# Three block programs of TensorE in another order, an early count and one wait less in a fused attention and mixture-of-experts kernel

## The chip, the cores and the metric

The kernel runs on one core of a Trainium2 chip. Its time is the time of one execution on the device in microseconds (us); where several runs are given, it is their median.

## What is computed

A chain of three parts on 3072 tokens (4 sequences of 768) with 512 features:

```python
# 1. decayed linear attention, 8 heads of 64, per sequence
state = gamma * state + outer(k[t], v[t]);  y[t] = scale * q[t] @ state
# 2. top-1 mixture of 8 experts, 512 -> 1024 -> 512
e_idx = argmax(x @ w_gate + modality_bias[modality_id])
out[mask] = gate_w[mask, None] * (relu(x[mask] @ w1[e]) @ w2[e])
# 3. bilinear part
h = (x @ w1) * (x @ w2) @ w3
result = h @ w_out
```

## The kernel before, in words

The program of each engine is written out by hand, and the engines meet through counting semaphores. Large products are made from a high and a low half of each operand: every product is three matmuls (helper on L400: high x high, high x low, low x high). ScalarE writes the high half, VectorE subtracts it from the source to get the low half.

There are three stages. The attention stage runs over 24 units (6 chunks of 128 rows in 4 sequences). Beside its end and behind it, w3 and w_out are multiplied into one matrix `wc` (eight products of 24 matmuls, `w3_product`), while VectorE sorts the tokens by expert into tiles of 128 places and writes small tables.

The expert stage works on blocks of one, three or four tiles of one expert. Each engine runs a loop of 13 passes (`each_window`): it loads the number of blocks from `num_tab` once, and in each pass compares it with the pass number; in a pass without a block it does nothing more. TensorE then loads the block's size from `win_tab` and runs one of three programs: `wide(4)` and `wide(3)` (8 hidden products of 12 matmuls, 4 outward products of 24, and two groups of 8 transposes of the next block's rows, with 512 or 384 columns) or `one_tile` (24 + 8 + 24 + 16 + 4 matmuls and transposes). Each program is in the code once. With this input there are eight blocks, of 4, 3, 3, 3, 4, 4, 4 and 1 tiles. POOL gathers the rows, SyncE loads the next expert's weights as soon as the present ones have been split.

`s_hlo` counts the low halves of the hidden layer that VectorE has written. A hidden product f of block w waits until it has reached 8w + f + 1, because its bank is free then. So that the first two products of block 0 may start, VectorE gives two counts by `dve.sem_inc(s_hlo, 2)` on L1383, behind the last piece of `wc` (`wc_lo(7)`) and just ahead of its own block loop. `s_wclo` counts the pieces of `wc` that are lowered; the banks of the outward products hold such pieces earlier.

The last stage, behind the loop, is six groups of 288 matmuls: two products with w1 and w2, and one with `wc`.

Of the kernel before, what the change touches and what calls it, by code (L numbers as in the profile page):

```python
# [32 lines left out]
def build(nc, q_t, k_t, k, v, mod_id, w_gate, mod_bias, we1, we2, wa, wb, w3_t, w_out, out):  # L33
# [9 lines left out]
    KF = FF // P  # L43
# [56 lines left out]
    with ctx:  # L100
# [127 lines left out]
        def sem(name):  # L228
            return ctx.enter_context(nc.semaphore(name))
# [48 lines left out]
        s_wclo = sem("s_wclo")  # L278
# [17 lines left out]
        s_hlo = sem("s_hlo")  # L296
# [48 lines left out]
        def each_window(eng, body):  # L345

            total = eng.value_load(num_tab[0:1, 1:2], min_val=MINW, max_val=NW)
            with eng.Fori(0, NW) as w:
                with eng.If(total > w):
                    body(w, total)  # L350

        def table(eng, w, col, lo, hi):

            at = win_tab[0:1, w:w + 1, col:col + 1] if isinstance(w, int) else win_tab[0:1, bass.ds(w, 1), col:col + 1]
            return eng.value_load(at.rearrange("p a b -> p (a b)"), min_val=lo, max_val=hi)  # L355
# [21 lines left out]
        def early_chunks(f):  # L377

            return (f - 3,) if 3 <= f < 3 + KD else ()
# [415 lines left out]
        def _(pe):  # L795
# [134 lines left out]
            def x_rows(w, chunks):  # L930
                pe.wait_ge(s_xin, w * (16 * GT) + 16 * GT)
                for k in chunks:
                    if not (isinstance(w, int) and w == 0):
                        pe.wait_ge(s_ixlo, w * KD + (k - 1))
                    for t in range(GT):
                        i = pe.transpose(bank[x_bank(w, k)][:, t * P:(t + 1) * P], xin[:, t, k * P:(k + 1) * P], ident)  # L936
                    i.then_inc(s_ixp, 1)

            def hidden(w, run, n, f):
                pe.wait_ge(s_hlo, w * KF + (f + 1))  # L940
                for k in range(KD):
                    if f == 0:
                        pe.wait_ge(s_ixlo, w * KD + (k + 1))
                        pe.wait_ge(s_w1lo, run * KD + (k + 1))
                    i = product(pe, bank[f % 2][:, 0:n], lambda a: we1_p[:, a, k, f * P:(f + 1) * P], lambda a: xT[:, a, k, 0:n],
                                k == 0, k == KD - 1)
                i.then_inc(s_hp, 1)

            def outward(w, run, n, d):
                pe.wait_ge(s_y, w * KD + (d + 1))  # L950
                for f in range(KF):
                    if d == 0:
                        pe.wait_ge(s_hlo, w * KF + (f + 3))
                        if f % 2 == 0:
                            pe.wait_ge(s_w2lo, run * (KF // 2) + (f // 2 + 1))
                    i = product(pe, bank[4 + d % 2][:, 0:n], lambda a: we2_p[:, a, f, d * P:(d + 1) * P], lambda a: hT[:, a, f, 0:n],
                                f == 0, f == KF - 1)
                i.then_inc(s_yp, 1)

            def window(w, total):  # L960
                def wide(tiles):
                    run = table(pe, w, RUN_OF, 0, E - 1)
                    n = tiles * P
                    for f in range(KF):
                        hidden(w, run, n, f)
                    for d in range(KD):
                        outward(w, run, n, d)
                        if d < KD // 2:
                            with pe.If(total > w + 1):
                                x_rows(w + 1, range(2 * d, 2 * d + 2))  # L970
# [29 lines left out]
                    i.then_inc(s_yp, KD - 1)  # L1000

                size = table(pe, w, SIZE, 1, GT)
                with pe.If(size > 3):
                    wide(4)
                with pe.If(size < 4):
                    with pe.If(size > 1):
                        wide(3)
                    with pe.If(size < 2):
                        one_tile()

            def first_x():
                x_rows(0, range(KD))
# [12 lines left out]
                if f == 3:  # L1025
                    token_of_place()
            pe.wait_ge(s_tab, 1)
            pe.wait_ge(s_wclo, KF - 2)
            each_window(pe, window)
            pe.wait_ge(s_wclo, KF)  # L1030

# [32 lines left out]
        def _(dve):  # L1064
# [23 lines left out]
            def lower(pair, raw, sm_):  # L1088
                tt(pair(LO), raw, pair(HI).bitcast(F32), ALU.subtract).then_inc(sm_, 1)  # L1089

            def w1_lo(run, chunks=range(KD)):
                for c in chunks:
                    dve.wait_ge(s_w1hi, run * KD + (c + 1))
                    lower(lambda a: we1_p[:, a, c, :], we1_raw[:, c, :], s_w1lo)
# [67 lines left out]
            def wc_lo(f):  # L1162
                dve.wait_ge(s_wchi, f + 1)
                tt(wc[:, LO, f, :], bank[wc_bank(f)][:, :], wc[:, HI, f, :].bitcast(F32), ALU.subtract).then_inc(s_wclo, 1)  # L1164
# [90 lines left out]
            wide = [1, E, E]  # L1255
# [7 lines left out]
            wide = [1, n_tab, E]  # L1263
# [42 lines left out]
            wide = [1, NG, n_tab]  # L1306
# [12 lines left out]
            w1_lo(0, early_chunks(4))  # L1319
            wc_lo(5)  # L1320
            w1_lo(0, early_chunks(5))
            wc_lo(6)
            w1_lo(0, early_chunks(6))
            x_lo(0, range(KD))
# [55 lines left out]
                with dve.If(total > w + 1):  # L1380
                    x_lo(w + 1, range(KD))

            dve.sem_inc(s_hlo, 2)  # L1383
            each_window(dve, window)


# [63 lines left out]
```

## Time and profile before

| | |
|---|---|
| median of three runs | 878.25 us |
| lowest, highest | 874.43, 881.44 us |
| profiled execution, its own time | 881.25 us |
| its span, first to last instruction | 879.5 us |
| mean granted clock of TensorE | 0.987 |
| TensorE busy in the span | 855.1 us |

The profiled execution's own time is 1.75 us longer than its span. Busy times of the other engines are far smaller (VectorE 283.7, ScalarE 236.2, POOL 89.5 us) and mostly lie beside TensorE's.

### The profile page before, as it was taken

The page shows a single profiled execution, that of the slowest core. Times are in us where ns is not written, and L with a number is a line of the kernel's source. Part 1 is how long each engine was busy: PE and PEld are TensorE (multiplying, and loading weights), DVE is VectorE, ACT ScalarE, POOL GpSimd, SP SyncE. Part 2 cuts the span into 40 slices and gives each one's busy share as a digit, 9 for nine tenths or more (in the row PEclk, how much of TensorE's full clock was granted, in tenths as well). Part 3 has the DMA queues.
Part 4 walks back from the last instruction along what each step waited for, and adds up shares of the span by engine and source line. Part 5 has one row for each costly group of instructions (what it writes and reads, how often), then busy time and mean ns, then how long its engine had stood idle before and what let it go on. Part 6 is the DMA issues. An engine that isn't in the chain of part 4 may idle for free.

```text
span 879.5 us, 14619 instructions
## 1 busy us (share of the span) xinstructions
PE 855.1 (97%) x5722; PEld 733.0 (83%) x5723; DVE 283.7 (32%) x493; ACT 236.2 (27%) x382; POOL 89.5 (10%) x111
## 2 busy tenths in 40 slices
PE   9999999998999999999987999999999999999995
PEld 8899888787999988888876888888888888888884
DVE  3577698521221432111414430230230220220210
ACT  1334433321222432121334331231221221221210
POOL 2222002210102020202000001001001001001001
PEclk9999999999999999999997999999999999999998
DMA  9999881432022042303045002002002001001000
GB/s 332 330 327 306 295 314 48 147 108 83 26 71 96 9 182 95 96 0 96 31 160 156 1 2 95 1 6 90 0 14 81 0 28 68 0 8 41 1 12 37
DMA packets 43093, 83.36 MB, mean 95 GB/s; under 512 B 7345, under 2 KB 7985, under 8 KB 43057
## 3 DMA queue, kind: packets, MB, share of 16 engines
q1 hardware_dynamic: 33376, 60.08, 20.0%
q0 software_dynamic: 4736, 14.72, 5.2%
q10 hardware_dynamic: 4946, 8.08, 2.5%
q8 instruction: 24, 0.39, 0.2%
q14 instruction: 11, 0.09, 0.0%
HBM read 62.64 MB, written 20.22 MB: 94 GB/s over the span
## 4 chain that ended last, share of the span: by engine, by line
PE 93%; DVE 3%; issue 2%; ACT 1%; ACTq 1%; POOL 0%; DVEq 0%
PE bank L400 46%; PE attn L400 33%; PE bank L831 3%; PE attn L858 3%; PE pair L843 3%; PE pair L936 1%; PE bank L870 1%; PE attn L849 1%; PE bank L808 1%; PE bank L1019 1%; DVE w3T L1089 0%; PE pair L815 0%; ACTq L355 0%; DVE wc L1164 0%; DVE we_p L1089 0%
## 5 line engine op out<-in xcount | busy, mean ns | idle before, releaser
L400 PE MATMUL bank<-yT,wab 128*128 128x512 f32 x1152 | 265.1, 392 | 3.4 <-issue 3.4
L400 PEld LDWEIGHTS bank<-yT,wab 128*128 128x128 f32 x1152 | 218.2, 190 | 49.2 <-issue 3.6
L400 PE MATMUL bank<-xT,we_p 128*128 128x512 f32 (+1 forms) x672 | 140.6, 370 | 4.9 <-issue 3.8
L400 PE MATMUL attn<-hT,we_p 128*128 128x512 f32 (+1 forms) x672 | 141.8, 368 | 0.0
L400 PEld LDWEIGHTS bank<-xT,we_p 128*128 128x128 f32 x672 | 123.3, 190 | 21.7 <-issue 6.2
L400 PEld LDWEIGHTS attn<-hT,we_p 128*128 128x128 f32 x672 | 121.3, 188 | 14.4
L400 PE MATMUL attn<-wc,gT 128*128 128x512 f32 x576 | 131.5, 389 | 0.0
L400 PEld LDWEIGHTS attn<-wc,gT 128*128 128x128 f32 x576 | 108.1, 188 | 22.5
L1390 DVE TENSOR_TENSOR g<-bank,acopy 128x512 f32<-128x512 f32 x48 | 33.2, 691 | 255.0 <-PE bank L400 255.0
L1335 DVE SCALAR_TENSOR_TENSOR hT<-bank,hT 128x512 fp32r<-128x512 f32 x56 | 38.7, 690 | 151.5 <-ACT hT L661 151.5
L587 ACT ACTIVATE gT<-g 128x512 fp32r<-128x512 f32 x48 | 30.3, 632 | 137.6 <-DVE g L1390 137.6
L661 ACT ACTIVATE hT<-bank 128x512 fp32r<-128x512 f32 x56 | 33.5, 599 | 103.0 <-PE bank L400 103.0
L574 POOL DMA_INDIRECT out_dram<-otile,row_id x24 | 23.2, 968 | 372.0 <-ACT otile L587 372.0
L587 ACT ACTIVATE acopy<-bank 128x512 f32<-128x512 f32 x48 | 28.7, 598 | 68.1 <-PE bank L400 68.1
L587 ACT ACTIVATE yout<-attn 128x512 f32<-128x512 f32 x29 | 17.3, 597 | 110.0 <-PE attn L400 109.2
L1089 DVE TENSOR_TENSOR gT<-g,gT 128x512 fp32r<-128x512 f32 x48 | 33.2, 692 | 34.4 <-ACT gT L587 34.4
L587 ACT ACTIVATE otile<-attn,meta_in 128x512 f32<-128x512 f32 x24 | 16.5, 689 | 100.0 <-PE attn L400 100.0
L1108 DVE TENSOR_TENSOR prob<-bank,maskt 128x512 f32<-128x512 f32 x48 | 30.9, 685 | 24.2 <-PE bank L831 24.1
L1089 DVE TENSOR_TENSOR xT<-pair,xT 128x512 fp32r<-128x512 f32 x30 | 19.3, 685 | 52.4 <-ACT xT L587 52.4
L1089 DVE TENSOR_TENSOR we_p<-we_raw,we_p 128x1024 fp32r<-128x1024 f32 x24 | 28.3, 1221 | 21.1 <-ACT we_p L587 20.9
L549 POOL DMA_INDIRECT xin<-x_rows,x_id x32 | 31.5, 984 | 11.1 <-issue 7.3
L587 ACT ACTIVATE xTu<-attn 128x512 f32<-128x512 f32 x24 | 14.4, 598 | 59.4 <-PE attn L858 59.4
(168 smaller groups left out, 609.2 us busy)
## 6 DMA issues: line engine op xcount, KB each, us to landing
we_raw<-in_moe_w_dram SPq DMA_DIRECT2D x6, 2048.0 KB, 8.9
yT_sorted<-yout ACTq DMA_DIRECT2D x7, 1024.0 KB, 4.4
qkv<-in_q_t_dram SPq DMA_DIRECT2D x24, 256.0 KB, 3.6
qkv<-in_v_dram SPq DMA_DIRECT2D x24, 256.0 KB, 5.0
x_rows<-x_keep SPq DMA_DIRECT2D x24, 256.0 KB, 3.6
ytile<-yT_sorted SPq DMA_DIRECT2D x6, 1024.0 KB, 5.3
qkv<-in_k_t_dram SPq DMA_DIRECT2D x23, 256.0 KB, 4.7
qkv<-in_k_dram SPq DMA_DIRECT2D x20, 256.0 KB, 5.2
```

Of the source, the lines that this page charges most:

```text
L400: i = pe.matmul(out_, left(a), right(b), start=(first and n == 0), stop=(last and n == 2), **kw)
L549: pool.indirect_dma_start(xin[:, t, :], None, x_rows[:, :], bass.IndirectOffsetOnAxis(ap=x_id[:, t:t + 1], axis=0)).then_inc(s_xin, 16)
L574: pool.indirect_dma_start(out[:, :], bass.IndirectOffsetOnAxis(ap=row_id[:, n:n + 1], axis=0), otile[:, n % 2, :], None).then_inc(s_out[n ...
L587: copy = lambda o, i, **kw: act.activation(o, i, ACT.Copy, **kw)
L661: act.activation(hT[:, HI, f, :], bank[f % 2][:, :], ACT.Relu).then_inc(s_hhi, 1)
L831: i = pe.matmul(bank[2 + r][halves(a), j * P:(j + 1) * P], qkv[head_rows(r), b, KT, keys], qkv[head_rows(r), b, QT, j * P:(j + 1) * P], st ...
L843: i = pe.matmul(pair[halves(a), j, 0:XW], xTu[:, b % 2, j, halves(a)], iw[:, j, :], start=True, stop=True, skip_group_check=True)
L858: i = pe.matmul(attn[out_rows(j, r), r, j // 2 * P:(j // 2 + 1) * P], qkv[:, b, V, h * D:(h + 1) * D], prob[:, b % 2, r, j, :], start=(fir ...
L1089: tt(pair(LO), raw, pair(HI).bitcast(F32), ALU.subtract).then_inc(sm_, 1)
L1108: i = tt(prob[:, u % 2, r, :, :], bank[2 + r][:, :].rearrange("p (j t) -> p j t", j=HP), maskt[:, r, :, :], ALU.mult)
L1335: dve.scalar_tensor_tensor(hT[:, LO, f, :], bank[f % 2][:, :], 0.0, hT[:, HI, f, :].bitcast(F32), ALU.max, ALU.subtract).then_inc(s_hlo, 1)
L1390: tt(g32[:, f % 2, :], bank[2 + f % 2][:, :], acopy[:, f % 2, :], ALU.mult).then_inc(s_g, 1)
```

## The change

Three edits. TensorE's three block programs stand in the code as one tile, three tiles, four tiles, where they stood as four, three, one. VectorE gives the two first counts of `s_hlo` behind the third early chunk of w1, ahead of `wc_lo(6)`. TensorE doesn't wait for six lowered pieces of `wc` ahead of its block loop. The instructions in each program are the same.

```diff
                 size = table(pe, w, SIZE, 1, GT)
+                with pe.If(size < 4):
+                    with pe.If(size < 2):
+                        one_tile()
+                    with pe.If(size > 1):
+                        wide(3)
                 with pe.If(size > 3):
                     wide(4)
-                with pe.If(size < 4):
-                    with pe.If(size > 1):
-                        wide(3)
-                    with pe.If(size < 2):
-                        one_tile()
...
             pe.wait_ge(s_tab, 1)
-            pe.wait_ge(s_wclo, KF - 2)
             each_window(pe, window)
...
             wc_lo(5)
             w1_lo(0, early_chunks(5))
+            dve.sem_inc(s_hlo, 2)
             wc_lo(6)
...
-            dve.sem_inc(s_hlo, 2)
             each_window(dve, window)
```

On TensorE, the entry of the block loop. Before, in program order; `num_tab` holds the number of blocks, `win_tab` the sizes, and the first COMPARE_AND_BRANCH of L1003 asks whether the size is above 3:

```order
L347 TENSOR_LOAD num_tab [waits s_wclo,s_tab]
L347 ISA x2
L348 UNCONDITIONAL_BRANCH
L349 COMPARE_AND_BRANCH
L355 ISA
L355 TENSOR_LOAD win_tab
L355 ISA x2
L1003 COMPARE_AND_BRANCH
...
L943 ISA [waits s_hlo]
L944 ISA [waits s_ixlo]
L400 MATMUL bank<-xT,we_p 128x512 [waits s_w1lo]
```

The same place in the changed kernel, where L1003 asks whether the size is below 4 and L1004 whether it is below 2:

```order
L347 TENSOR_LOAD num_tab [waits s_tab]
...
L355 TENSOR_LOAD win_tab
L355 ISA x2
L1003 COMPARE_AND_BRANCH
L1004 COMPARE_AND_BRANCH
...
L977 ISA [waits s_hlo]
L978 ISA [waits s_ixlo]
L400 MATMUL bank<-we_p,xT 128x512 [waits s_w1lo]
```

Straight behind the compares stood the four-tile program; now the one-tile program stands there, and a block of four tiles branches at L1003 over it and over the three-tile program.

On TensorE, the end of the four-tile program. Before, with the start of the three-tile program behind it:

```order
L400 MATMUL attn<-hT,we_p 128x512 [waits s_y]
L400 MATMUL attn<-hT,we_p 128x512 x23
L1003 UNCONDITIONAL_BRANCH
L1005 COMPARE_AND_BRANCH
L1006 COMPARE_AND_BRANCH
```

In the changed kernel, with the back edge of the loop and the first matmul of the last stage behind it:

```order
L400 MATMUL attn<-hT,we_p 128x512 [waits s_y]
L400 MATMUL attn<-hT,we_p 128x512 x23
L348 REGISTER_ALU
L348 COMPARE_AND_BRANCH
L400 MATMUL bank<-yT,wab 128x512 [waits s_yTlo,s_walo,s_wclo]
```

The four-tile program was followed by the other two; now it is the last one, and the loop's end stands right behind it. The programs of 208 + 76 matmuls between them are passed at another place.

## Rows read from the trace of the kernel before

**Rows 1.** The page: span, and TensorE's busy time and share.
```profile
span 879.5 us, 14619 instructions
...
PE 855.1 (97%) x5722; PEld 733.0 (83%) x5723; DVE 283.7 (32%) x493; ACT 236.2 (27%) x382; POOL 89.5 (10%) x111
```

**Rows 2.** Waits of PE: who waited for whom, us in total, times, longest.
```profile
PE bank L400 <- issue: 7.2, 3, 3.5
...
PE bank L400 <- DVEq L1383: 0.9, 1, 0.9
```

**Rows 3.** The chain in 148 to 165: start us, us, what.
```profile
158.56 0.04 DVE wc L1164
...
158.83 6.18 PE bank L400 x26
```

**Rows 4.** Timeline, 139 to 186, VectorE and SyncE: start, us, engine, operation.
```profile
151.95 0.68 DVE L1164 TENSOR_TENSOR wc<-attn,wc 128x512 fp32r<-128x512 f32 x1
...
152.55 1.21 DVE L1089 TENSOR_TENSOR we_p<-we_raw,we_p 128x1024 fp32r<-128x1024 f32 x1
...
155.67 0.39 SPq L469 DMA_DIRECT2D we_raw<-in_moe_w_dram  x1
...
156.61 1.28 DVE L1089 TENSOR_TENSOR xT<-pair,xT 128x512 fp32r<-128x512 f32 x2
```

**Rows 5.** Timeline of PE where blocks 1, 2, 4 and the last stage begin.
```profile
207.95 8.25 PE L400 MATMUL bank<-xT,we_p 128*128 128x384 f32 x37 [3.53 <-issue]
...
245.12 1.14 PE L400 MATMUL bank<-xT,we_p 128*128 128x384 f32 x5 [0.28 <-issue]
...
316.25 1.09 PE L400 MATMUL bank<-xT,we_p 128*128 128x512 f32 x4
...
475.20 6.99 PE L400 MATMUL bank<-yT,wab 128*128 128x512 f32 x17 [3.35 <-issue]
```

**Rows 6.** The page's DMA queues: packets, MB, share of 16 engines.
```profile
q8 instruction: 24, 0.39, 0.2%
```

**Rows 7.** Queues in stretches from 163.2, 201.3, 204.8, 242.8, 525.6, 553.8, 0.2 us each.
```profile
q8 instruction: 1, 0.02, 30.0%
...
q8 instruction: 1, 0.02, 39.3%
...
q8 instruction: 1, 0.02, 31.6%
...
q8 instruction: 1, 0.02, 41.3%
...
q8 instruction: 1, 0.02, 44.2%
...
q8 instruction: 1, 0.02, 39.0%
```

**Rows 8.** Queues in 243 to 480: the only one of kind instruction.
```profile
q14 instruction: 1, 0.01, 0.0%
```

**Rows 9.** The chain in 200 to 209.
```profile
199.89 4.53 PE attn L400 x20
```

**Rows 10.** Windows: stretch, length, busy us of each engine, PEclk, DMA share, GB/s.
```profile
0.00:50.00 50.00, 47.89 (x924) 44.01 (x927) 24.45 (x55) 11.66 (x20) 13.03 (x21) 1.00 0.94 330
...
155.00:158.00 3.00, 2.90 (x13) 2.06 (x11) 2.89 (x5) 0.07 (x1) 2.39 (x3) 1.00 0.42 63
158.00:165.00 7.00, 6.17 (x27) 5.14 (x28) 1.38 (x2) 1.53 (x3) 2.82 (x4) 1.00 1.01 409
...
207.95:211.60 3.65, 3.65 (x12) 3.65 (x13) 0.00 (x0) 0.00 (x0) 0.00 (x0) 0.54 0.25 95
...
475.20:481.20 6.00, 6.00 (x14) 4.74 (x15) 1.46 (x2) 0.46 (x2) 1.15 (x1) 0.50 0.59 160
```

**Rows 11.** Timeline of PE in the attention stage, at two breaks.
```profile
35.76 0.55 PE L831 MATMUL bank<-qkv 64*64 64x128 f32 x10 [0.20 <-issue]
...
41.07 1.09 PE L858 MATMUL attn<-prob,qkv 128*64 128x128 f32 x16 [0.33 <-issue]
```

## The prediction

> **What bounds the kernel now.** The page comes first: TensorE (PE) is busy 855.1 of 879.5 us [rows 1]. So only PE's idle time, and time at a low clock, can change the end. The table of waits says where PE is idle: 7.2 us in three pieces put down to "issue" (nothing that the profile shows), and 0.9 us put down to VectorE's semaphore instruction on L1383 [rows 2]. The reader should see that the change touches exactly these: L1383 is the early count that is moved, and two of the three issue pieces stand at the block programs whose order is changed.
>
> The place of the 0.9 us: the last w3 product ends at 157.9, ScalarE copies its bank, VectorE starts the subtraction at 158.56, and only then issues the count; PE starts block 0 at 158.83 [rows 3], 0.9 us after its last matmul. The wait that is removed (six wc pieces lowered) was long met: the sixth subtraction of wc began at 151.95 and took 0.68 us [rows 4].
>
> The issue pieces: reading PE's rows at the borders of the eight blocks, block 1 (three tiles) starts at 207.95 after 3.53 us of issue, block 2 (three tiles) after 0.28 us, and block 4 (four tiles) with none; blocks 3, 5, 6 and 7 are like block 4 [rows 5]. 475.20 is the start of the last stage, 3.35 us after the loop. So a three-tile program costs 3.53 us the first time and next to nothing the second. What differs is that its code was new to PE. The transfers of kind "instruction" say the same: the queue q8 moved 24 packets of 0.39 MB in all, 16 KB each [rows 6]. One lies at 201.3 to 201.5 and one at 204.8 to 205.0, around the 3.53 us; from 243 to 480, through five blocks and the exit, q8 moves nothing at all, and the one row of that kind is q14's [rows 7, 8]. I read this as: code comes in pieces of 16 KB, the next piece is fetched ahead while PE goes straight on, a jump to a piece that isn't there waits for its transfer, and pieces once fetched stay for this loop.
>
> How much is a piece? In the last stage, straight-line code, packets start at 525.6 and 553.8 [rows 7]. With 4.53 us for 20 matmuls [rows 9], 0.227 us each, 28.2 us is 124 matmuls with their weight loads. By the code, the four-tile and the three-tile program have 208 matmuls each (96 + 96 and 16 transposes) (1.7 pieces), the one-tile program 76 (0.6). In the kernel before, PE runs the four-tile program straight through, then skips the three-tile and the one-tile programs, 2.3 pieces, to the loop's end: the first such jump lands beyond the piece fetched ahead. That is the stall at 204.42.
>
> **The change, part by part.** All sums are against the profiled execution, 881.25 us for a span of 879.5; the median of the three runs is 878.25, and I carry the difference over to it.
>
> Removed at the first border: with the order one tile, three tiles, four tiles, the end of the four-tile program is followed by the loop's end, and the piece after it is fetched ahead. Block 1 then jumps back to the head and skips only the one-tile program, 0.6 of a piece, which was fetched ahead when PE came to the head. The stall of 3.53 us goes. With it goes a slow stretch: the granted clock is 0.54 over the 3.65 us behind the idle time, nearly all of it at 1.2 GHz [rows 10]; 0.46 x 3.65 is 1.7 us. Together 5.2 us. What is late next there: the path from one block to the next, which the borders after it show as 0.28 us or hidden.
>
> Added at the entry: block 0 has four tiles. PE's sequencer now passes the head, finds size above 3 and jumps over the one-tile and three-tile programs, 2.3 pieces, to code that nobody has fetched. The same kind of stall as at 204.42 is due here, with the same sort of matmul (512 columns) running ahead of it. Its price has four parts. The row of it, 3.53 us. The entry also loads the number of blocks, ahead of the jump: a border without a fetch takes at least from 242.8, where the sequencer is at the loop's end, to the start at 245.12, 2.3 us, for two table loads and the branches; less one empty pass (3.35 us for five at the exit, 0.67; the loop has 13 passes for 8 blocks) leaves 0.8 per load; some of it stands against the back edge that the entry doesn't have, so I take 0.4, between 0 and 0.8. Third, the DMA engines: at 201 they were nearly free, and the two packets there stand 3.5 us apart; in the attention stage, with the engines busy 94% [rows 10], PE came to a fresh piece at 35.76 and again at 41.07, each time after a short issue gap in the middle of its straight-line work [rows 11], so a fetch took up to 5.3 us there, 1.8 more. At the entry the DMA share is 0.42 in 155 to 158 and 1.01 after 158, when the weights of the second expert run stream in; I take 0.7, between 0 and 1.8. The stall is 4.6 us (3.5 to 6.1), and block 0 starts near 162.5. Fourth, the clock: 1.7 us again by the nearest row; the exit's stall was followed by 6.0 us at 0.50, worth 3.0 [rows 10], which is the upper bound.
>
> The early count: VectorE gives it behind the third chunk of w1, which starts at 152.55 and takes 1.21 [rows 4], so from 153.8 on. VectorE spends nothing on it, and nothing queues behind it. The 0.93 us disappear as a wait on VectorE, but the gain is real only to the extent that the new stall does not cover it; I count the stall from 157.90, so 0.93 is taken off whole. Other counts that PE needs (w1 chunks, x pieces) are in by 157.9, the end of the last two x pieces [rows 4]. The removed wait: nothing, as shown; under a fetch of code it could only matter if PE's sequencer had come before 152.6. The PE path at the exit: block 7 has one tile, and its program now stands first, so two more compares are passed before the loop's end; five empty passes of at least three such instructions cost 0.67 each, so two compares are at most 0.4 and I take 0.2. They are not hidden, since PE is idle there. The four-tile blocks pass one branch less, within the lead.
>
> Sum: 4.6 + 1.7 + 0.2 - 0.93 - 3.53 - 1.7 = +0.3 us. The stall changes its place and hardly its size. Bounds: +0.3 - 1.1 - 0.2 = -1.0 and +0.3 + 1.5 + 1.3 + 0.2 = +3.3. That gives 881.6 for an execution like the profiled one and **878.6** against the median.
>
> **Rivals.**
> Hidden fetch: the four-tile program is there when PE jumps, or comes while the w3 products still run. For it: PE's sequencer is some microseconds ahead of its array (the packet at 201.3 begins 3 us before the last matmul of block 0 ends). Against it: the same lead stood before the stall of 3.53 us and did not hide it. It gives -0.93 - 3.53 - 1.7 + 0.2 = -6.0, so 872.3. Chance 10%.
>
> Late fetch, the slower side: the new fetch queues behind the 2 MB of expert weights that are issued at 155.67 [rows 4]. For it: the code packet of block 0 in the kernel before starts only at 163.2 [rows 7], in the middle of that load. If the demanded piece starts there too: at the border PE resumed 6.5 us after the packet's start (201.4 to 207.95), of which the head's branches and the size load, some 2 us by the prices above, lie ahead of the jump here. So PE resumes near 163.3 + 4.5 = 167.8, a stall of 9.9 instead of 4.6: +5.3, so 883.9. It decides against the kernel once the packet starts later than about 157.7, where the stall is 4.3 us. Against it: PE should be at the jump near 156, and the engines are half free until 158. Chance 12%.
>
> Both stalls: the piece with the head or the three-tile program is lost, and the border at block 1 stalls as before. That adds 5.2 to the sum, so 883.8. Against it: the head's piece survived the fetches up to 242.8 in the kernel before [rows 7], since block 2 came back to it for 0.28 us. The Trainium skill has a rule that leads here (Runtime: NRT & Kernel Launch, Instruction fetch mechanics): a taken branch whose target isn't in the current two pages of 16 KB forces a fetch. By that rule every border, in both kernels, would stall; the trace does not agree, with 0.28 us at 245.12, nothing at 316.25, and no code packet in 237 us [rows 5, 8]. Chance 5%.
>
> Not code at all: the 3.53 us belong to something that the order of the programs doesn't touch. Then only the early count acts, at most -0.9, so 877.4. The two packets beside the stall speak against it. Chance 5%.
>
> **How the numbers follow.** The forecast has 68%; its own range, with the bounds above and the spread of a median (the three runs lie 7 us apart), is 875 to 882.5. The range for 8 in 10 reaches half into the cases on each side: 873.5 to 883.5. A measurement of this kernel tells about 1%, 8.8 us, from no change. No single case moves that far: late fetch and both stalls together would. So faster 0.02, within 1% 0.94, slower 0.04.
>
> **What would show it.** In the changed profile: PE idle of 3.5 to 6 us put down to issue ahead of the first matmul of block 0, near 162; a code packet near 157 to 158.5; a clock near one half behind it; no idle of 3.5 us ahead of block 1; the wait on VectorE's count gone from the table; the idle time of the exit at 3.4 to 3.7 us. Block 0 starting by 158 proves the hidden fetch; a start past 165 proves the late one.

## The result, and the profile after

| | before | changed |
|---|---|---|
| median, 20 runs of each | 878.49 us | 882.96 us |
| lowest, highest | 874.34, 881.44 us | 880.32, 887.05 us |
| profiled execution, its own time | 881.25 us | 882.88 us |
| its span | 879.5 us | 881.2 us |

The ratio is 1.0055 with a 95% interval of 1.0042 to 1.0069. The changed kernel is 4.5 us slower, between 3.7 and 6.1. The time lies in the range given for 8 in 10 (873.5 to 883.5) and within 1% of before, but above 882.5, where the forecast case itself ended. The likeliest time was 878.6, and the missing 4.4 us are no chance: the interval leaves the ratio 1 out.

The page of the changed kernel, to be read against [rows 1, 6]: span, busy times and the queue of kind instruction.

```profile
span 881.2 us, 14618 instructions
...
PE 853.3 (97%) x5722; PEld 732.3 (83%) x5723; DVE 283.9 (32%) x493; ACT 236.1 (27%) x382; POOL 88.5 (10%) x111
...
q8 instruction: 26, 0.43, 0.2%
```

There are 26 code packets, two more than before. The waits of PE, against [rows 2]:

```profile
PE bank L400 <- issue: 7.2, 2, 4.4
...
PE bank L400 <- DVE wab L1088: 3.9, 1, 3.9
```

The count's wait on VectorE is gone. The sum put down to issue is 7.2 us again, which looks like no change, but it is now two pieces and the exit's idle time stands in the other row: before, 7.2 was 3.53 + 0.28 + 3.35. The exit's row names VectorE's piece of `wab`, but PE doesn't wait for it: that piece ends 3.67 us behind the last block's end in both traces, and before PE had started at 3.35. Where the pieces stand, on the timeline of PE (against [rows 5]):

```profile
160.34 23.68 PE L400 MATMUL bank<-xT,we_p 128*128 128x512 f32 x96 [2.86 <-issue]
...
207.41 4.35 PE L400 MATMUL bank<-xT,we_p 128*128 128x384 f32 x24
212.24 12.78 PE L400 MATMUL bank<-xT,we_p 128*128 128x384 f32 x72 [0.48 <-DVE hT L1335]
...
247.83 19.23 PE L400 MATMUL bank<-xT,we_p 128*128 128x384 f32 x96 [4.38 <-issue]
```

The same matmuls of blocks 0, 1 and 2 before:

```profile
158.83 22.05 PE L400 MATMUL bank<-xT,we_p 128*128 128x512 f32 x96 [0.93 <-DVEq L1383]
...
207.95 18.47 PE L400 MATMUL bank<-xT,we_p 128*128 128x384 f32 x96 [3.53 <-issue]
...
245.12 17.09 PE L400 MATMUL bank<-xT,we_p 128*128 128x384 f32 x96 [0.28 <-issue]
```

Block 0 starts after 2.86 us, block 1 with none (before: 3.53), and block 2 after 4.38 us (before: 0.28). The 0.48 us inside block 1 are new too: ScalarE comes from a four-tile block, its copy `hT` lies at 210.86, and VectorE and PE follow it.

That these are waits for code can be read from the records of PE's sequencer (the part of the engine that reads the code and hands the matmuls on). The compare-and-branch instructions of the block programs, first before (L1005), then in the changed kernel (L1003 at the entry, L1008 ahead of block 2), with shortest, median and longest time in ns:

```profile
L1005 PEldq COMPARE_BRANCH  x2: 73/2030/3988, 200.2 to 206.1; - x2
```
```profile
L1003 PEldq COMPARE_BRANCH  x1: 3800/3800/3800, 155.2 to 155.2; - x1
...
L1008 PEldq COMPARE_BRANCH  x1: 3896/3896/3896, 240.2 to 240.2; - x1
```

One branch takes 4.0 us before, and two take 3.8 and 3.9 us in the changed kernel; no other branch of PE takes over 0.35 us in either. Each of the three is a jump over programs that aren't run, and each stands ahead of one of the three stalls (3.53, 2.86 and 4.38 us).

Windows behind the two stalls, with the columns of [rows 10]:

```profile
160.34:164.50 4.16, 4.16 (x11) 3.33 (x12) 0.00 (x0) 0.00 (x0) 0.80 (x1) 0.59 1.02 407
...
243.44:247.83 4.39, 0.01 (x2) 0.01 (x1) 0.00 (x0) 0.60 (x1) 0.00 (x0) 0.80 0.63 173
247.83:251.50 3.67, 3.67 (x11) 3.67 (x12) 0.00 (x0) 0.00 (x0) 0.00 (x0) 0.50 0.23 86
251.50:254.00 2.50, 2.50 (x12) 2.50 (x12) 0.69 (x1) 0.60 (x1) 0.00 (x0) 0.73 0.00 0
```

The number behind the five busy times of a row is the granted clock. Behind the entry it is 0.59 over 4.16 us, by the clock alone 0.41 x 4.16 = 1.7 us; behind block 2's stall it is 0.50 and then 0.73, 1.8 + 0.7 = 2.5 us. The matmuls themselves lost a little less: the first 96 of block 0 took 23.68 us against 22.05 (1.6), those of block 2 took 19.23 against 17.09 (2.1), and those of block 1 before took 1.4 more than those of block 2. The stalls of code stand beside packets. Queues in stretches from 155.9 (0.3 us long), 241.7 (0.2) and 246.8 (0.3), against [rows 7]; a packet is counted in the stretch in which it starts, and its share gives how long it took, 0.306 x 16 x 0.3 = 1.47 us for the first:

```profile
q8 instruction: 1, 0.02, 30.6%
...
q8 instruction: 1, 0.02, 30.2%
...
q8 instruction: 1, 0.02, 24.0%
```

They start at 156.17, 241.74 and 246.93 and take 1.47, 0.96 and 1.15 us. The first two lie inside the two long branches (155.22 to 159.02 and 240.18 to 244.07). The third isn't over when PE's matmuls go on at 247.83, so block 2 didn't wait for it. Before, the two last packets of the block loop started at 231.9 and 242.9, and no stall of over 0.3 us stood beside them.

The sum of the two profiled spans, +1.7 us, goes so: attention and w3 stages -0.4; entry +1.9 idle and +1.6 clock; border of block 1 -3.53, -1.4 clock and +0.48; border of block 2 +4.1 idle (4.38 - 0.28) and +2.1 clock; exit +0.57; the one-tile block -2.6 and the last stage -1.3; the rest +0.2. The one-tile block's term is put down to this pair of executions and not to the change: the clock fell there in this one of the kernel before, and didn't in this one of the changed kernel. The same holds for the last stage, where the granted clock over the first 6 us was 0.50 before [rows 10] and 0.72 after. The stretches from the last block's start to its end, before and then after:

```profile
452.21:471.85 19.64, 15.80 (x61) 11.91 (x59) 10.69 (x12) 11.27 (x16) 0.00 (x0) 0.83 0.40 145
```
```profile
457.23:474.26 17.03, 13.15 (x61) 10.00 (x59) 9.80 (x12) 11.19 (x16) 0.00 (x0) 1.00 0.31 109
```

Without those two the spans differ by +5.6 us, against +4.5 between the medians.

### The profile page after: what moved, and what is told of

Its sections match the earlier page's. It is cut to its first block, busy times and chain, and to the rows that moved or that the text cites. A ratio compares the mean times of both kernels' runs of the same rounds, so it can differ in the third digit from the quotient of the medians.

```text
span 881.2 us, 14618 instructions
## 1 busy us (share of the span) xinstructions
PE 853.3 (97%) x5722; PEld 732.3 (83%) x5723; DVE 283.9 (32%) x493; ACT 236.1 (27%) x382; POOL 88.5 (10%) x111
## 4 chain that ended last, share of the span: by engine, by line
PE 92%; DVE 3%; issue 2%; ACT 1%; ACTq 1%; POOL 0%; DVEq 0%
PE bank L400 46%; PE attn L400 32%; PE bank L831 3%; PE attn L858 3%; PE pair L843 3%; PE pair L936 1%; PE bank L870 1%; PE attn L849 1%; PE bank L808 1%; ACTq L355 1%; PE bank L1019 1%; DVE w3T L1088 0%; PE pair L815 0%; ACT wab L587 0%; ACT yout L587 0%
## 5 line engine op out<-in xcount | busy, mean ns | idle before, releaser
L400 PE MATMUL bank<-xT,we_p 128*128 128x512 f32 (+1 forms) x672 | 143.1, 374 | 7.9 <-issue 7.2
L400 PEld LDWEIGHTS bank<-xT,we_p 128*128 128x128 f32 x672 | 125.3, 193 | 25.2 <-issue 8.6
```

Of the source, the lines that this page charges most:

```text
L400: i = pe.matmul(out_, left(a), right(b), start=(first and n == 0), stop=(last and n == 2), **kw)
```

## The experiments

Two theories stood against each other. **The hole** (mine, formed from the result) supposes this: PE's code comes in pieces of 16 KB, some 256 instructions, and the next piece is fetched ahead when PE enters a new one. A jump to a piece that wasn't asked for stalls and leaves the pieces between unfetched. When PE later runs through them, they are fetched, and those behind them once more; if PE then jumps again before a piece is back, it stalls a second time. **The rival**: the second stall belongs to something else in the changed kernel (the early count, the missing wait, the data path from a four-tile to a three-tile block), or to where the programs stand in sequence, whatever the pieces.

Counted in the built programs, in pieces of 256 instructions, the positions are these:

```
                 loop's head   programs in order                   loop's end
before           9.95          four -11.72, three -13.50, one      14.20
changed          9.95          one -10.65, three -12.42, four      14.19
```

At the entry the changed kernel jumps from 9.95 to 12.42. By the theory piece 11 has not been fetched, nor asked for. Block 1 then runs through 10 and 11 and jumps from 12.42 to the end in 14: that is the border of the 4.38 us.

The stages of each profiled execution in us, as far as they matter here ("entry" is the idle time ahead of block 0, "exit" that ahead of the last stage, "q8" the number of code packets, "border" the largest idle time of PE put down to issue ahead of block 1 or 2). The ratio is to the kernel before, run beside it on the same chip, with its 95% interval; the medians come from more than one chip. The experiments have 4 (e8) to 12 runs each.

| run | median us | ratio | entry | border | exit | q8 |
|---|---|---|---|---|---|---|
| before | 878.49 | | 0.93 | 3.53, block 1 | 3.35 | 24 |
| changed | 882.96 | 1.0055 (1.0042 to 1.0069) | 2.86 | 4.38, block 2 | 3.92 | 26 |
| e1 order alone | 882.41 | 1.0054 (1.0033 to 1.0075) | 2.61 | 4.97, block 2 | 3.88 | 26 |
| e2 count alone | 877.32 | 0.9993 (0.9982 to 1.0005) | 0 | 3.55, block 1 | 3.40 | 24 |
| e3 three, four, one | 876.74 | 0.9978 (0.9963 to 0.9993) | 2.64 | none | 3.39 | 22 |
| e4 60 increments | 877.60 | 0.9990 (0.9973 to 1.0007) | 2.72 | none | 3.91 | 22 |
| e5 one, four, three | 878.60 | 1.0004 (0.9992 to 1.0016) | 0 | 3.06, block 1 | 3.61 | 22 |
| e6 the same, 186 increments | 880.33 | 1.0030 (1.0013 to 1.0048) | 0 | none | 3.66 | 22 |
| e7 10 increments | 884.08 | 1.0063 (1.0045 to 1.0081) | 2.92 | 5.03, block 2 | 3.87 | 26 |
| e8 20 increments | 884.53 | 1.0076 (1.0052 to 1.0101) | 2.40 | 4.84, block 2 | 4.89 | 26 |
| e9 three, four, one, skip | 873.47 | 0.9949 (0.9927 to 0.9972) | 0 | none | 3.35 | 22 |
| e10 one, four, three, skip | 873.35 | 0.9950 (0.9932 to 0.9968) | 0 | none | 3.66 | 22 |
| e11 40 increments | 876.75 | 0.9990 (0.9974 to 1.0006) | 2.80 | none | 3.87 | 22 |
| e12 e9, count late | 875.03 | 0.9964 (0.9951 to 0.9977) | 0.93 | none | 3.35 | 22 |

"None" stands for less than 0.3 us. The records of PE's sequencer agree with the table row by row: there are 14 branches of 3.3 to 4.5 us in all, one for each stall of over 2 us in the columns "entry" and "border", each with one code packet starting inside it, and no other branch of PE in any of these runs takes over 0.46 us.

**The order alone** (e1): the changed kernel, with the early count and the missing wait undone.

```diff
             pe.wait_ge(s_tab, 1)
+            pe.wait_ge(s_wclo, KF - 2)
...
-            dve.sem_inc(s_hlo, 2)
             wc_lo(6)
...
+            dve.sem_inc(s_hlo, 2)
             each_window(dve, window)
```

> The order of the three programs is changed, the early count and the wait stay as in the kernel before. Theory: the order alone makes the loss. The stall ahead of block 0 ends with the fetch of code (block 0 starts near 160.3), later than VectorE's count at its old place (158.2), so the count and the wait are worth nothing beside it: 882.5 to 883.5 us, stalls put down to issue of about 2.9 us at the entry and 4.4 us ahead of block 2, 26 code packets on q8. Rival: the early count or the removed wait lets the sequencer run into the fetch at another time, and the second stall comes from there: then this kernel is near 878 to 880 and has no stall ahead of block 2.

It has both stalls, 26 packets and the time of the changed kernel. The timeline of PE, where block 0's 96 matmuls take 22.05 us: behind this stall of the entry the clock didn't fall.

```profile
157.99 22.05 PE L400 MATMUL bank<-xT,we_p 128*128 128x512 f32 x96 [2.61 <-issue]
...
244.40 7.93 PE L400 MATMUL bank<-xT,we_p 128*128 128x384 f32 x33 [4.97 <-issue]
```

The loss is the order's. Beside it the early count is worth nothing behind a stall that is longer than its wait, and the removed wait is worth nothing.

**The count alone** (e2): the kernel before, with the count given early.

```diff
             w1_lo(0, early_chunks(5))
+            dve.sem_inc(s_hlo, 2)
...
-            dve.sem_inc(s_hlo, 2)
             each_window(dve, window)
```

> The order of the kernel before, with VectorE's early count alone. Theory: the sequencer is ahead of the array, so the count was the last thing that block 0 waited for; the 0.9 us of idle time there fall to 0 to 0.3 us, and the time is 0.5 to 0.9 us below the kernel before, 877.6 to 878.0. The stall of 3.5 us ahead of block 1 stays, with 24 code packets. Rival: the table loads end at the same time as the count, then the idle time stays 0.6 us or more, put down to issue, and the time is that of the kernel before.

The 0.93 us of idle time are gone, and the border of block 1 has its 3.55 us as before. The median is 0.7 us lower; the interval reaches from -1.6 to +0.4, so the time alone doesn't show it.

**Another order** (e3): three, four, one, with the other two edits kept. The entry jumps from 9.95 to 11.72, with piece 10 there: it lands in a piece that isn't there, but leaves none out. The four-tile program now ends at 13.49 and jumps into piece 14, the next one. The edit against the kernel before:

```diff
                 size = table(pe, w, SIZE, 1, GT)
-                with pe.If(size > 3):
-                    wide(4)
                 with pe.If(size < 4):
                     with pe.If(size > 1):
                         wide(3)
-                    with pe.If(size < 2):
-                        one_tile()
+                with pe.If(size > 3):
+                    wide(4)
+                with pe.If(size < 2):
+                    one_tile()
```

> The changed kernel with the programs in the order three, four, one tile. Counted in the code, in pieces of 256 instructions from the piece that begins at the attention stage's break: the head of the loop is at 9.95, three tiles 9.95 to 11.72, four tiles to 13.49, one tile to 14.19. Theory (hole): a fetched piece is put behind the piece that asked for it, so code fetched beyond a gap is thrown out when the gap is filled. Here the entry jumps to 11.72 with piece 10 fetched: one stall at the entry (about 2.9 us and 1.7 us of low clock) and no gap. No stall at any border after that, 22 code packets, and against the kernel before -0.9 -3.5 -1.7 +2.9 +1.7 = -1.5 us, so about 877. Rival (first jump): any jump beyond the next piece stalls the first time that it is taken, whatever was fetched: then the first end of a three-tile block (11.72 to 14.19) stalls too, ahead of block 2, 4.4 us and 1.8 us of clock: about 883.

There are 22 packets, the entry's stall as in the changed kernel, and no other:

```profile
161.55 24.95 PE L400 MATMUL bank<-xT,we_p 128*128 128x512 f32 x96 [2.64 <-issue]
...
214.71 12.75 PE L400 MATMUL bank<-xT,we_p 128*128 128x384 f32 x72 [0.48 <-DVE hT L1335]
```

Here block 0's 96 matmuls take 24.95 us, 2.9 more than in e1 behind a stall of the same size. This profiled execution was the slowest of the 12 (882.04 us against the median of 876.74).

The 0.48 us inside block 1 stay, so they belong to the meeting of a four-tile and a three-tile block once PE comes to it without a stall; in the kernel before the 3.53 us covered them.

**Where the pieces' borders lie** (e4): the changed kernel, with 60 increments of a semaphore in PE's program ahead of the loop. The order and the data stay; the loop moves 60 instructions on, so that its head lies in piece 10.

```diff
             for f in range(1, KF):
+                for _ in range(10 if f in (2, 3, 4, 5, 6, 7) else 0):
+                    pe.sem_inc(s_begun, 1)
                 w3_product(f, ...)
```

> The changed kernel as it is, with 60 increments of a semaphore that nobody waits for on TensorE, 10 ahead of each of the last six w3 products. They shift the block loop by 60 instructions against the pieces: the head comes to lie at 10.18, so that piece 11 is fetched by the time that the entry jumps to the four-tile program at 12.66. Theory (hole): the entry still stalls for piece 12 (2.5 to 3.5 us), but no gap is left; the stall of 4.4 us ahead of block 2 and its 2.4 us of low clock are gone, 22 code packets instead of 26, and the time is 5.5 to 6.5 us below the changed kernel, 876.5 to 877.5. Rival (first jump): the jump from the end of the three-tile program (12.65) to the loop's end (14.43) is still new, so the stall ahead of block 2 stays and the time is 883 or, with the cost of the 60 instructions, up to 886.

The second stall is gone: 22 packets, and 877.60 us against 882.41 of e1, which ran beside it on the same chip. The order is that of the changed kernel, so the rival that asks only for the sequence of the programs is out. What the 60 executed increments do besides moving the code is the question of e7, e8 and e11.

**One, four, three** (e5), the four-tile program in the middle: a short jump at the entry, and one at the end of block 0 over the three-tile program. The new order's lines, the old one's left out:

```diff
+                with pe.If(size < 2):
+                    one_tile()
+                with pe.If(size > 1):
+                    with pe.If(size > 3):
+                        wide(4)
+                    with pe.If(size < 4):
+                        wide(3)
```

> The changed kernel with the programs in the order one, four, three tiles, the last two inside one question (size above 1), so that the exit behind a one-tile block passes one compare more than in the kernel before. Nothing is shifted. In pieces: head 9.95, one tile to 10.64, four tiles 10.65 to 12.42, three tiles to 14.19. Theory (hole): the entry jumps into piece 10, which is there: no stall at the entry, and no idle time there with the early count. The end of block 0 jumps from 12.42 to 14.19 with piece 13 asked for and 14 not: one stall of 3.5 us ahead of block 1 with 1.7 us of low clock, no gap, 22 code packets. Against the kernel before -0.7 +0.25: 877 to 878.5. Rival (first jump): the first jump of the entry over the one-tile program stalls as well, +2.9 and +1.7, near 882.

No stall at the entry (block 0 follows the w3 product with no idle time), and 3.06 us at block 1. The entry's jump to 10.65 lands in the next piece and is free. The four-tile program ends at 12.42 and the jump lands in piece 14, with 13 asked for: a stall, but no piece left out, and 22 packets.

**The same, moved by 186 increments** (e6), so that the jump at the end of block 0 lands in the piece behind the present one.

```diff
+                for _ in range(31 if f in (2, 3, 4, 5, 6, 7) else 0):
+                    pe.sem_inc(s_begun, 1)
                 w3_product(f, ...)
```

> The kernel one, four, three with 186 increments of a semaphore that nobody waits for, 31 ahead of each of the last six w3 products. They shift the four-tile program's end to 13.15 and the loop's end to 14.93, into the piece behind it. Theory (hole): no jump of the block loop goes to a piece that isn't asked for in time; no stall put down to issue at the entry or at any border (0.3 us at most), 22 code packets, and against the kernel before -0.7 -3.5 -1.7 +0.5 +0.25 = -5.2 us: 872 to 874. This would be the fastest of all. Rival (price of the padding): 186 instructions of some 40 ns each, 7 us in all, come out of the sequencer's lead and show as idle time in the w3 products: 876 or more.

The stall is gone, but the increments cost more than it did. They hold up the w3 products, and the waits that follow show it:

```profile
137.49 12.74 PE L400 MATMUL attn<-w_out_p,w3T 128*128 128x512 f32 x48 [2.67 <-DVE w3T L1090]
150.86 5.69 PE L400 MATMUL bank<-w_out_p,w3T 128*128 128x512 f32 x24 [0.63 <-issue]
157.21 1.62 PE L400 MATMUL bank<-w_out_p,w3T 128*128 128x512 f32 x6 [0.66 <-issue]
```

The w3 stage takes 60.8 us where it took 54.3 in e5, 6.5 us more: PE is idle for 5.0 us in it (0.5 in e5), and the clock is at one half for 3.4 us. The rival to the gain, a loss by the padding, was right. It is no fixed price of an increment: with the 60 of e4 the stage takes 54.3 us as well. That the first increments hide in the sequencer's lead is likely, but no run was made for it.

**How far the loop must move** (e7 and e8): 10 and 20 increments instead of 60. With 10, the entry's compare is four instructions ahead of piece 10; with 20 it is six into that piece.

```diff
+                for _ in range(10 if f in (5,) else 0):       # e8: f in (5, 6)
+                    pe.sem_inc(s_begun, 1)
                 w3_product(f, ...)
```

> The changed kernel with 10 increments of a semaphore that nobody waits for ahead of the fifth w3 product. The compare that jumps over the other programs comes to lie at instruction 2751, four instructions before piece 10 begins (2755). Theory (hole): nothing changes against the changed kernel: stall at the entry and 4.4 to 5 us ahead of block 2, 26 code packets, 882 to 884. Rival (the padding itself, by delay or by giving the sequencer something to do, took the second stall away in the run with 60): some of the 4.4 us is gone here.

> The same with 20 increments, ahead of the fifth and sixth w3 products. The compare comes to lie at 2761, in piece 10, so the sequencer has asked for piece 11 when it jumps to piece 12. Theory (hole): ten instructions more than in the run before take away the whole second stall: idle only at the entry, none ahead of block 2, 22 code packets, 876.5 to 878. Rival (the padding itself): like the run with 10, or a small part of the way to the run with 60.

e7 keeps the second stall, as the hole has it. So does e8, 4.84 us and 26 packets, where I had expected none. So 10 or 20 increments by themselves don't take the stall away, and whether the compare lies in the new piece is not what decides. The windows of e8 around its stall:

```profile
240.56:245.40 4.84, 0.01 (x1) 0.01 (x1) 0.00 (x0) 0.60 (x1) 0.00 (x0) 0.80 0.63 208
245.40:249.20 3.80, 3.80 (x12) 3.80 (x13) 0.00 (x0) 0.00 (x0) 0.00 (x0) 0.50 0.05 17
```

**In between** (e11): 40 increments, the compare 26 instructions into piece 10.

```diff
+                for _ in range(10 if f in (4, 5, 6, 7) else 0):
+                    pe.sem_inc(s_begun, 1)
                 w3_product(f, ...)
```

> The changed kernel with 40 increments. The compare that jumps lies at 2781, 26 instructions into piece 10, where it was 6 in the run with 20 and 46 in the run with 60. Theory: what counts is that piece 11 has been asked for early enough (a packet starts 1.4 us or so after the piece before is entered) and not only that the jump lies in piece 10; 26 instructions are 7 matmuls of the last product, 1.6 us, and two table loads, some 3 us. So no gap: no stall ahead of block 2, 22 code packets, 877 to 878.5. Rival: the padding acts by its number of instructions, 60 being enough: then 40 is like 20, a stall of 4.8 us ahead of block 2, 26 packets, 884.

22 packets and no second stall. The timeline of PE at the border of block 2, where e8 stands still for 4.84 us:

```profile
239.68 3.98 PE L400 MATMUL attn<-hT,we_p 128*128 128x384 f32 x22
243.69 17.35 PE L400 MATMUL bank<-xT,we_p 128*128 128x384 f32 x96
```

Its packets near the entry start at 153.4 and 156.55, where e8 has one, at 155.4; behind the entry, e11 has three up to 194.6 and then none before 490, and e8 has eight up to 243.5. The long branch starts at 155.5 in e11, so its first packet came ahead of the jump; in e8 it starts at 154.45, ahead of the only one. I read it so: in e11 the next piece (11) was asked for before the jump's own, and in e8 it wasn't, although PE had entered piece 10. The request of the next piece must go out before the jump; six instructions are too few for that, 26 are enough. The changed order was not run with increments that are skipped, so that the 40 and 60 executed ones act by position alone is read from these packets.

**Both stalls avoided at no price** (e9 and e10). The orders of e3 and e5, moved by 50 and 181 increments that PE skips: it branches over them on a zero that it loads. The extra instructions around them count too.

```diff
             for f in range(1, KF):
+                if f == 2:
+                    pe.wait_ge(s_const, 16)
+                    nothing = pe.value_load(ident[0:1, 1:2].bitcast(I32), min_val=0, max_val=1)
+                    with pe.If(nothing > 0):
+                        for _ in range(50):                  # e10: 181
+                            pe.sem_inc(s_begun, 1)
                 w3_product(f, ...)
```

> The kernel three, four, one tile, shifted by 55 instructions that TensorE doesn't run: ahead of the third w3 product it loads a zero from the constants and skips a block of 50 increments. In pieces: head 10.14 to 10.16, three tiles to 11.94, four tiles 11.94 to 13.71, one tile to 14.41. Theory (hole, and a piece is asked for when the piece before it is entered): piece 11 is asked for some 36 instructions ahead of the jump to 11.94, piece 14 while block 0 is in piece 13. No stall at the entry (under 0.3 us) or at any border, the exit as in the kernel before (3.4 us), 22 code packets, and 5.2 to 5.8 us below the kernel before: near 872.5. Rival (too late): piece 11 is asked for, but the jump comes before it is usable: a rest of 0.5 to 2.5 us of idle time at the entry, 873.5 to 876.

> The kernel one, four, three tiles, shifted by 186 instructions as the one with 186 increments, but now 181 of them are skipped as in the run before. Theory: the loss of the padded one, a w3 stage of 60.8 us where it was 54.3, came from running the increments. Here that stage is 54.3 again, no stall at the entry or a border, exit 3.6 us, 22 code packets: 872 to 873.5. Rival: the shift itself costs (another border of pieces in the w3 products, or the skip of 181 instructions lands in a piece that isn't there): the w3 stage is 56 us or longer.

In e9 the entry's jump lands at 11.9, with piece 11 asked for since PE entered piece 10. Both are 0.5% faster than the kernel before (873.47 and 873.35 against 878.5), and so faster than the changed one too. In e10 the w3 stage takes 54.3 us, with 181 increments skipped where e6 ran 186. In e9 PE goes from the w3 product into block 0, from there into block 1, and the clock stays whole. Timeline and a window:

```profile
151.93 4.34 PE L400 MATMUL bank<-w_out_p,w3T 128*128 128x512 f32 x18
156.11 22.25 PE L400 MATMUL bank<-xT,we_p 128*128 128x512 f32 x96
...
201.74 4.35 PE L400 MATMUL bank<-xT,we_p 128*128 128x384 f32 x24
```
```profile
157.00:160.00 3.00, 2.96 (x13) 2.15 (x12) 0.65 (x2) 0.60 (x1) 1.98 (x4) 1.00 1.02 403
```

**The count's worth without the stalls** (e12): e9 with the count given late and the wait kept.

```diff
             pe.wait_ge(s_tab, 1)
+            pe.wait_ge(s_wclo, KF - 2)
...
-            dve.sem_inc(s_hlo, 2)
             wc_lo(6)
...
+            dve.sem_inc(s_hlo, 2)
             each_window(dve, window)
```

> The kernel of the first of these four with the count at its old place and the wait for six pieces of wc kept. Theory: with no stall at the entry the count is the last thing that block 0 waits for again: 0.9 us of idle time put down to VectorE's count, and the time 0.7 to 1.1 us above the first of these four. Rival: the count is worth nothing, the same time within 0.2 us.

The 0.93 us are back on the timeline of PE, put down to VectorE's count, and the median is 1.6 us above e9's, more than the 0.7 to 1.1 expected, though the two intervals overlap.

```profile
158.83 22.05 PE L400 MATMUL bank<-xT,we_p 128*128 128x512 f32 x96 [0.93 <-DVEq L1389]
```

## Why the prediction was right and wrong

- **The stall of the first border goes: right.** Block 1 starts with none, and with no clock loss behind it: 3.53 us and, by the length of the matmuls, 1.4 of clock, 4.9 where 5.2 stood. What is late next there was said to be the path that later borders show; it was ScalarE's copy, 0.48 us.
- **The added stall at the entry: right in its place and kind, too large.** 2.86 us (2.4 to 2.9 in seven kernels) where 4.6 stood and 3.5 was the low end. The mistake is in taking over the row of 3.53 us, which is a sum of its own. At block 1 before, the branch holds the sequencer for 3.99 us, its way back to the head and through the table loads takes another 3.76 until the first matmul, and its lead over the last matmul takes off 4.22. At the entry the branch takes 3.80, what is behind it 1.32, since the head has been passed, and the lead takes off 2.27. The 0.4 for the table's load was therefore no addition. The term of 0.7 for busy DMA engines was at most 0.2: the packet took 1.47 us against 1.26. The 5.3 us that bounded it were no fetch: the packets of the attention stage up to 44 us took 0.9 to 1.8 us. The packets that the prediction read as "201.3 to 201.5" and "204.8 to 205.0" only start there and take 1.26 and 1.01 us. The rival late fetch rested on a packet at 163.2; in the changed kernel the packet inside the branch starts at 156.17, and the next, at 162.19, is the like of that one.
- **The clock behind the entry: right here, in part by luck.** The nearest row gave 1.7 us and the matmuls lost 1.6. But behind stalls of the same kind, 2.4 to 2.9 us, the same 96 matmuls took 22.05 us in e1 and e8 (no loss), 23.7 in e7 and e11, and 24.9 in e3 and e4 (2.9 us).
- **The failing step** is the sum's account of the borders. "Pieces once fetched stay for this loop" was read off the blocks from 243 to 480 and taken for all; the entry's jump over 2.5 pieces had a further consequence at a border where the kernel before showed 0.28 us. Missed were 4.1 us of idle time and 2.1 of clock ahead of block 2, 6.2 us in all. The rival "both stalls" named the like of it, a piece that is lost, and priced it at +5.2 and a chance of 5%; it set it at block 1, where it did not come. The row that spoke against it, the head's survival up to 242.8, was right about the head: the branch that waits ahead of block 2 is the one to the loop's end. e4 and e11 show that the stall hangs on where the code lies, e1 that the order brings it. That the time still fell into the wide range is owed in part to the entry's stall, put 1.7 us too high.
- The number of packets bears the hole out. Where no jump leaves a piece out (e3 to e6, e9 to e12) there are 22. Before, the jump at the end of block 0 goes from 11.72 to 14.20, with 12 asked for: piece 13 is left out, and there are 24. In the changed kernel the entry leaves 11 out, with more pieces already fetched behind it, and there are 26. So the second fetch of a piece stood in the kernel before too [rows 6], where it came in time to be hidden; how many pieces its code has was a count that the prediction didn't make. The long branches of 3.8 and 3.9 us agree with a rule of the Trainium skill (Runtime: NRT & Kernel Launch, Instruction fetch mechanics), by which a taken branch outside two pages forces a fetch. The later borders don't, with 237 us without a packet [rows 8].
- **The early count** takes away its 0.93 us of idle time where no stall covers it (e2, e12) and nothing behind one (e1 against the changed kernel). Its term was subtracted whole, which was right, since the 2.86 us are counted from the last w3 matmul as the 4.6 were. **The removed wait**: nothing, as forecast.
- **The exit's two compares** cost 0.57 us (3.92 - 3.35; 0.52 to 0.57 in the kernels of this order, e8 apart with 4.89), where 0.2 was taken and 0.4 was the upper bound. They are passed once, 0.27 us each by the records of PE's sequencer; e5, e6 and e10, with one compare more, show 0.26 to 0.31. The bound had come from a mean over empty passes.

With the measured terms: 2.86 + 1.6 + 0.57 - 0.93 - 3.53 - 1.4 + 0.48 + 4.1 + 2.1 = +5.9 us, and +5.5 with the 0.4 that the stages ahead of it gave; the medians say +4.5 (3.7 to 6.1).

**What stays open.** No trace names the piece that a packet brings, so which pieces are dropped or fetched again is inferred from positions, packet counts and stalls. Where between 6 and 26 instructions ahead of a jump the request of the next piece leaves was not tried. Why e8's exit took 4.89 us, 1 us more than its like, is open too: no code packet stands there, and its five empty passes took 0.94 us each on average where those of the changed kernel took 0.74. Why the clock fell behind some of the entry's stalls and not behind others wasn't tested.

## What to carry to other kernels

Where the bound engine runs one of several long programs in a loop, the order of the programs sets which jumps land in code that isn't there, and a gap left by one jump can be paid for at another. Look for compare-and-branch records of PE that take microseconds, at its idle time put down to issue, and at the packets of kind instruction, and count them: more packets than the code has pieces mean that some are fetched twice. Move such a jump until it lands at most one piece ahead and some instructions behind the start of a piece, and put a long filling where it is skipped and not run: 186 executed increments gave the gain back, 181 skipped ones kept all 5 us.

## What the runs showed of the hardware

- A branch of PE into code that isn't there took 3.3 to 4.5 us (14 of them in ten kernels), and the code packet inside it 0.9 to 2.0 us. PE's matmuls stood still for 2.4 to 5.0 us: that time, plus the sequencer's way to the next matmul (1.3 us at the entry and 3.8 at a border of these two kernels), less its lead (2.3 and 3.3 in the changed kernel, 4.2 at block 1 before).
- Behind the changed kernel's stalls of 2.86 and 4.38 us the granted clock was near one half (0.59 over 4.2 us, 0.50 over 3.7 us; the 1.2 GHz level), and the matmuls took 1.6 and 2.1 us longer. Behind the entry's stall of 2.4 to 2.9 us the loss was anything from 0 to 2.9 us.
- A shift of 40 or 60 instructions made the changed kernel 6 and 5 us faster (e11, e4), and one of 10 or 20 did nothing for it (e7, e8).
- 60 increments of a semaphore spread over PE's w3 products cost nothing that shows (54.3 us, e4), 186 cost 6.5 us (60.8 us, e6).
- A compare that PE passes while its array is idle costs about 0.27 us (the two at the exit of the changed kernel).
